# Attention over 48 heads: a deeper software pipeline, a fourth buffer for q and k, half of v's split on another engine

## The reference

```python
def rmsnorm(x, g):
    return x / np.sqrt(np.mean(x * x, axis=-1, keepdims=True) + 1e-06) * g
# q, k, v: (4, 12, 448, 64) float32
scores = (1 / sqrt(64)) * rmsnorm(q, g_q) @ rmsnorm(k, g_k).T      # 448 x 448, for each of 48 heads
attn = exp(scores - max); attn /= attn.sum() + 1e-9
x = (attn @ v) as (1792, 768)
# then: top-1 routing of the 1792 rows over 8 experts (cosine logits / tau),
# two matmuls per expert (768 -> 1024 -> 768), and a dense feed-forward 768 -> 2048 -> 768
```

## Time and profile before

| | us |
|---|---|
| three runs, median | 1331.34 |
| the profiled execution, its own time | 1328.66 |
| its span on the core | 1326.9 |
| attention: start to the first row sums of routing | 0 to 386 |
| of it the fill, up to the first head's `copy_u` | 34.9 |
| of it 48 heads, first to last `copy_u` | 348.1 |
| routing | 386 to 408 |
| experts and feed-forward | 408 to 1326.9 |

### The profile page before, as it was taken

The page is one execution under the profiler, slowest core; times in us unless marked ns, Lnnn a source line. Parts: engine busy times, 40 slices in busy tenths (PEclk is TensorE's granted clock), DMA queues, the critical chain, the costliest instruction groups (busy, mean ns, idle before and its releaser), DMA issues. The chain is left out here.

```text
span 1326.9 us, 21193 instructions
## 1 busy us (share of the span) xinstructions
PE 1232.0 (93%) x6986; PEld 1072.3 (81%) x6986; DVE 891.8 (67%) x1305; ACT 751.0 (57%) x1434; POOL 529.2 (40%) x533
## 2 busy tenths in 40 slices
PE   5988999999955999999999995999999999999998
PEld 3766777777744889998899985899999999999997
DVE  4877888888874999999999994455432235552222
ACT  4888888888873878777787774322241122221111
POOL 6666767676713776677766661000000000000000
PEclk9999999999986999999999997899999999999999
DMA  1233233322201355555555104121132222211222
GB/s 49 67 94 96 84 93 94 92 59 70 58 15 36 120 225 190 185 191 190 192 215 184 61 24 133 46 60 49 63 111 58 86 72 69 73 51 44 57 87 71
DMA packets 99979, 126.45 MB, mean 95 GB/s; under 512 B 28568, under 2 KB 81048, under 8 KB 99872
## 3 DMA queue, kind: packets, MB, share of 16 engines
q1 hardware_dynamic: 92416, 103.07, 25.6%
q0 software_dynamic: 3360, 16.52, 3.4%
q10 hardware_dynamic: 4096, 5.51, 1.2%
HBM read 193.88 MB, written 19.27 MB: 161 GB/s over the span
## 5 line engine op out<-in xcount | busy, mean ns | idle before, releaser
L1017 ACT CAST w_hi<-w_raw 128x768 fp32r<-128x768 f32 (+1 forms) x294 | 249.4, 930 | 15.2 <-DMA w_raw<-moe_w_in 13.9
L1087 DVE TENSOR_TENSOR w_lo<-w_raw,w_hi 128x1024 fp32r<-128x1024 f32 x84 | 187.9, 2272 | 9.7 <-POOL w_lo L906 7.0
L408 DVE TENSOR_TENSOR pT_lo<-ps_pt,pT_hi 112x448 fp32r<-112x448 f32 x192 | 115.1, 620 | 66.5 <-ACT pT_hi L354 66.3
L345 ACT ACTIVATE probs<-ps_s,neg_max 112x448 f32<-112x448 f32 x192 | 124.4, 648 | 45.1 <-DVE neg_max L402 45.1
L1497 DVE TENSOR_TENSOR out_lo<-out_raw,out_hi 128x384 fp32r<-128x384 f32 x64 | 35.7, 558 | 169.4 <-ACT out_hi L1406 169.4
L1288 PE MATMUL ps_acc<-yT_hi,in_hi 128*128 128x448 f32 x384 | 142.5, 371 | 2.1 <-DVE yT_lo L1483 2.1
L1318 PE MATMUL ps_acc<-gT_hi,out_hi 128*128 128x448 f32 x384 | 142.5, 371 | 0.0
L906 POOL TENSOR_TENSOR w_lo<-w_raw,w_hi 128x1024 fp32r<-128x1024 f32 x42 | 105.2, 2505 | 93.0 <-ACT w_hi L1017 93.0
L1289 PE MATMUL ps_acc<-yT_hi,in_lo 128*128 128x448 f32 x384 | 141.5, 369 | 0.0
L1290 PE MATMUL ps_acc<-yT_lo,in_hi 128*128 128x448 f32 x384 | 141.4, 368 | 0.0
L1320 PE MATMUL ps_acc<-gT_lo,out_hi 128*128 128x448 f32 x384 | 140.4, 366 | 0.0
(11 more groups left out here) (184 smaller groups left out, 2935.0 us busy)
## 6 DMA issues: line engine op xcount, KB each, us to landing
w_raw<-moe_w_in SPq DMA_DIRECT2D x84, 1536.0 KB
in_raw<-moe_w_in_in SPq DMA_DIRECT2D x32, 384.0 KB, 3.3
out_raw<-moe_w_out_in SPq DMA_DIRECT2D x64, 192.0 KB, 2.4
qk_raw<-q_in SPq DMA_DIRECT2D x48, 112.0 KB, 2.8
qk_raw<-k_in SPq DMA_DIRECT2D x48, 112.0 KB, 2.8
v_raw<-v_in SPq DMA_DIRECT2D x48, 112.0 KB, 2.0
x_rows<-x_tok SPq DMA_DIRECT2D x48, 112.0 KB, 2.5
out_rows<-o_sb ACTq DMA_DIRECT2D x26, 168.0 KB, 2.4
```

The lines of the kernel that those rows point to most:

```text
L345: act.activation(probs[:, t, :], ps_s[0:R, t, 0:S], ACT.Exp, bias=neg_max[u][:, t:t + 1], accum_out=sums[u][:, t:t + 1]).then_inc(s_exp, 1)
L1017: act.copy(out[:, c, :], raw[:, c, :]).then_inc(s_hi, 1)
L1087: dve.tensor_tensor(w1_lo[:, c, :], w1_raw[:, c, :], w1_hi[:, c, :].bitcast(F32), ALU.subtract).then_inc(s_w1lo, 1)
```

## The change

- The orders of the loops of PE, ACT, DVE and POOL are new, and each loop mixes steps of more heads. PE's iteration m now starts with transpose_p 1 (m) and runs values (m-1) on either side of transpose_p 2 (m); transposes of q are for head m+2, of k for m+3, scores g1 for m+1, g0 for m+2. ACT squares head m+4, POOL folds head m+5.
- `qk_raw` has four buffers instead of three: q and k of head n wait for the norms of head n-4.
- `v` of head n is issued by SP behind q and k of head n+5, and the store of head n behind q and k of head n+9 (LAG 9, V_LAG 5).
- The high part of v is made by POOL (`high_v`, a tensor_copy) instead of ACT. It comes first in POOL's iteration; `guard_sums` and `fold_squares` stand between it and the low part. `norm_q` and `norm_k` of a head now come one iteration after its `invert_rms`.
- `mix` holds 12 blocks instead of 48 (heads of the four batches share them), so that the copies that fill it once at the start are shorter.

The core of the diff:

```diff
-    LAG = 6
+    LAG = 9
+    V_LAG = 5
...
-        qk_raw = [sb(f"qk_raw{w}", [R, 2, T, D]) for w in range(3)]
+        qk_raw = [sb(f"qk_raw{w}", [R, 2, T, D]) for w in range(4)]
...
-        mix = sb("mix", [P, N, X])
+        mix = sb("mix", [P, H, X])
...
+            def load_qk(n):
+
+                if n > 3:
+                    sp.wait_ge(s_qn, n - 3)
+                    sp.wait_ge(s_kn, n - 3)
...
+            def load_v(n):
                 if n > 1:
                     sp.wait_ge(s_vhl, n - 1)
...
+            def step(n):
+                if n < N:
+                    load_qk(n)
+                if 2 <= n - V_LAG < N:
+                    load_v(n - V_LAG)
+                if 0 <= n - LAG < N:
+                    store(n - LAG)
...
+            def high_v(n, u):
+                pool.wait_ge(s_v_in[u], fills(n, u, 16))
+                if n > 1:
+                    pool.wait_ge(s_u, n - 1)
+                pool.tensor_copy(v_hl[u][:, :, 0, :], v_raw[u][:, :, :]).then_inc(s_vhi, 1)
```

More of the change, by code:

```diff
@@ L79, in attention @@
         s_gain_in, s_gain = sem("s_gain_in"), sem("s_gain")
-        s_qk_in = [sem(f"s_qk_in{w}") for w in range(3)]
+        s_qk_in = [sem(f"s_qk_in{w}") for w in range(4)]
         s_v_in = [sem(f"s_v_in{u}") for u in range(2)]
@@ L107, in store @@
                 sp.dma_start(x_dest[:, :, bass.ds(n * D, D)], x_tok[:, :, bass.ds(n, 1), 0:D].rearrange("p t o d -> p t (o d)")).then_inc(s_x_out, 16)
[L109 to L120, removed]
+            def step(n):
[5 more added lines that the diff above has]
+                    store(n - LAG)
+            load_qk(0)
             for half in range(2):
@@ L123, in _ @@
                     sp.dma_start(gains[half * D:(half + 1) * D, i:i + 1], g.rearrange("(d o) -> d o", o=1)).then_inc(s_gain_in, 16)
-            load(1, 1)
+            load_qk(1)
             sp.dma_start(emb_sb[:, :], emb).then_inc(s_emb, 16)
             sp.dma_start(tau_b[:, :], tau.rearrange("(o t) -> o t", o=1).to_broadcast([E, 1])).then_inc(s_emb, 16)
[L127 to L134, removed]
+            for n in range(2, 4):
+                load_qk(n)
+            load_v(0)
+            load_v(1)
+            for n in range(4, N + LAG):
+                step(n)
+                if LAG < n <= LAG + 2 * (C1 + C2) and (n - LAG) % 2 == 0:
+                    c = (n - LAG) // 2 - 1
+                    w, raw = (w1, w1_raw[:, c, :]) if c < C1 else (w2, w2_raw[:, c - C1, :])
+                    c = c if c < C1 else c - C1
+                    sp.dma_start(raw, w[0, c * P:(c + 1) * P, :]).then_inc(s_first, 16)
         def fills(n, u, per):
@@ L278, in transpose_emb @@
                     last.then_inc(s_te, 1)
[L280 to L289, removed]
+            for m in range(-3, N + 1):
                 if 0 <= m < N:
                     transpose_p(m, m % 2, 1)
+                if 0 <= m - 1 < N:
+                    values(m - 1, (m - 1) % 2, 0)
+                if 0 <= m < N:
                     transpose_p(m, m % 2, 2)
+                if 0 <= m - 1 < N:
+                    values(m - 1, (m - 1) % 2, 1)
+                if 0 <= m + 2 < N:
+                    transpose_q(m + 2, (m + 2) % 2)
                 if 0 <= m + 1 < N:
-                    scores(m + 1, (m + 1) % 2, 0)
-                if m + 2 < N:
-                    transpose_k(m + 2, (m + 2) % 2)
+                    scores(m + 1, (m + 1) % 2, 1)
                 if 0 <= m < N:
@@ L299, in _ @@
                     transpose_p(m, m % 2, 3)
-                if m - 1 >= 0:
+                if 0 <= m + 1 < N:
+                    transpose_p(m + 1, (m + 1) % 2, 0)
+                if 0 <= m - 1 < N:
                     outputs(m - 1, (m - 1) % 2)
+                if 0 <= m + 3 < N:
+                    transpose_k(m + 3, (m + 3) % 2)
+                if 0 <= m + 2 < N:
+                    scores(m + 2, (m + 2) % 2, 0)
         @block.scalar
@@ L373, in _ @@
                 if 0 <= m + 1 < N:
[L374 to L379, removed]
-                    copy_q(m + 1, (m + 1) % 2)
[L381 to L387, removed]
+                    copy_q(m + 1, (m + 1) % 2)
+                if 0 <= m - 2 < N:
+                    copy_u(m - 2, (m - 2) % 2)
         @block.vector
```

100 lines of the change are left out of this document (45 added, 55 removed).

## The result

The changed kernel takes 1275.22 us (median of four runs, 1275.01 to 1277.84) against 1331.46 of the kernel before in its four. The ratio is 0.9584, 95% interval 0.9562 to 0.9605: 56 us less. The forecast was 1290, with 1277 as its low end, so the mechanism and the sign were right and the gain was sized at 38 us instead of 54 on the profiled execution. That execution's own time is 1275.01 us, its span 1273.3. One run in this document, of the kernel before with the fourth buffer and v behind q and k, took 1725.86 us at a granted clock of 0.654, where the five others of that kernel had 0.971 to 0.976, and is left out of its number.

A forecast was written before the change was run, and what follows sets the result against it. A ring of waits between ACT and DVE was taken to bound attention. New attention 307.2 us less 348.1 now, plus 2.4 for fill, gives -38.5 on 1328.66: 1290.2, given as 1290; range 1277 to 1312.

The forecast's parts named there:

- The next bound is PE's list itself: Attention loop: under the new orders no ring through ACT and DVE is as long as PE's own work, 6.55 us a head.
- 6.55 us for that list, and 6.6 a head: PE in attention: work summed from start distances to 6.56, taken as 6.55, plus 0.05 us for small waits.
- Each change costs a tenth more or less: PE: uncertainty per change between transposes and products, giving 6.4 to 6.7 us a head.
- The ring of the kernel before: Attention: ACT and DVE wait for each other through low part 1 and row maxima, setting 7.36 us a head.
- v on POOL: High part of v: ACT loses 0.41 us a head, POOL gains a copy of 0.45 (0.20 to 0.74); zero price.
- q and k four heads ahead: Loads with the fourth buffer: the square's stall goes; priced nothing, at worst the 0.05 us a head remains.
- Fill: Start of attention up to the first `copy_u`: 37.3 instead of 34.9 us, +2.4, with 0 and +6 as ends.
- Drain: End of attention: last two iterations lack steps of heads that do not exist; 10.2 us up to the last `copy_u`.
- (1): Attention: ring shorter but not gone, 6.8 to 7.2 us a head, 1299 to 1317; chance 0.19.
- (2): Attention: PE has less work than its spacing says and DVE binds, 6.1 us a head, 1268; chance 0.07.
- (3): Attention: POOL binds from a copy of 1.4 us; 1344 at 2.6; chance 0.07 including other ways of losing.
- (4): No change within 0.3%: PE keeps waits of 0.8 us a head, for example for `ps_pt`; chance 0.05.

The follow-up runs named there:

- A shorter list: Changed kernel without the product of v with the low part of the probabilities (half of PE's matmuls of values): 1252.73 us, ratio 0.9431.
- the three orders: Changed kernel, on PE: outputs and k's transposes exchanged, 1276.89 us; transposes 1 and 2 side by side, 1279.48; q's beside them too, with DVE exchange, 1279.55.
- the runs with v on POOL: Kernel before with v's high part on POOL: 1327.96 us; the same plus fourth buffer and v issued behind q and k of three heads later: 1322.72.
- the runs above: Kernel before with fourth buffer and v issued behind q and k of three heads later: 1324.56 us, ratio 0.9952; with the buffer alone: 1329.74, 0.9997.

## Why the prediction was right and wrong, point by point

- **"The next bound is PE's list itself"**: right. A shorter list makes attention shorter by 23.8 us, and PE is busy in 200.00 of 200 us, which alone would not show it. The plan's waits came as written down: ACT waits for PE's transposes 2 (31 times, up to 0.4 us; 0.6 was read) and for nobody else.
- **6.55 us for that list, and 6.6 a head**: this is the step that failed, a term sized too long in a mechanism that was right. Measured is 6.39, in four orders 6.38 to 6.39. The 6.56 was pieced together from start distances of one early head of the kernel before; the head shown above adds up to 6.40. Of the 0.16 between them 0.07 is a step priced by its likeness: the last part of the probabilities was taken at 0.44, as the transposes of k, and is 0.37 ahead of values (204.41 to 204.78). Another 0.05 are the two halves of values, 0.93 and 0.91 there, 0.90 and 0.89 here. The other steps differ by their neighbours, up and down: outputs 0.85 ahead of scores and 0.75 ahead of k, q 0.12 ahead of values and 0.28 ahead of scores. Why the old head's distances came out longer stays open; waits too short to be listed are likely, and aren't shown. With 0.05 on top for waits that didn't come it is 45 x 0.21 = 9.4 us. These alone would have given 1281, still in the range.
- **"Each change costs a tenth more or less"** as the bound of that term: wrong in kind, as the three orders show. It was the reason for 6.4 as a low end, where 6.4 was the value.
- **The ring of the kernel before**: it is there, but the claim that ACT's and DVE's handovers alone set 7.36 was incomplete. A second ring through PE had the same length, and the runs with v on POOL show it. For the forecast it made no difference, as the plan of the new order was checked against every wait in the code, not against the one ring.
- **v on POOL**: the copy is 0.405 us, in the range of 0.20 to 0.74 and near the 0.45 taken:

```profile
L153 POOL CAST v_hl<-v_raw 112x256 fp32r<-112x256 f32 x32 | 13.0, 405 | 0.0
```

  From start to start it costs 0.35 here (203.40 to 203.75 in the trace of the changed kernel). The advice of the Trainium skill (GPSIMD Engine Reference, Engine selection) against elementwise work on that engine has no weight in the new order: with the copy on ACT or on POOL attention takes the same time.
- **q and k four heads ahead**: the stall is gone as said, no square waits in full pipeline. The prediction saw in the buffer the 2.3 us of late heads, net of the drain (the runs above give 5 to 6); in the new order its absence costs 24.8. The forecast's sum doesn't change by it, but whoever ranks the parts of the change by that price leaves out the one that carries it.
- **Fill**: +2.4 us was forecast, +0.2 came (35.1 against 34.9). PE was taken at its lower speed up to iteration 1. The scores of the new fill show it at full speed from 25.4 on, 0.53 and then 0.36 for matmuls of the same shape, where before it came at 31.7. k of head 3 was there about when it was said (its transposes start at 30.28, 29.7 was put down), but iteration 1 starts at 31.87 and not at 34.5. Why the speed rose earlier isn't shown: from 17 to 25 us PE is busy 6.62 us in the new fill and 6.38 in the old.

```profile
25.07 0.53 PE L232 MATMUL ps_s<-kT_lo,qT_hi 64*112 64x448 f32 x2
25.44 0.36 PE L232 MATMUL ps_s<-kT_hi,qT_lo 64*112 64x448 f32 x2
```

- **Drain**: the last heads take 5.68, 5.07 and 4.05 us from copy to copy, 1.8 us less than was put down.
- **The sum of the misses**: 9.4 for the list and the waits, 1.8 for the drain, 2.2 for the fill, 1.7 behind attention: 15.1 of 1290.2 - 1275.0 = 15.2 us. The range missed by 1.8 us: with 6.4 a head it had 1281 and 4 us below that, and the other three, 5.7 us in sum, all went the same way. The last of them lies within what traces of the same code differ by (942.9 to 946.2 in the other kernels of the document), so that much is luck.
- **The rivals**: (1) no ring was left. (2) PE's list was indeed shorter than its spacing said, by 0.16 and not by 0.5. By the Trainium skill's rule on weight loads (Perfetto Trace Analysis, Identifying the Most-Contended Engine) PE would have had room: weight loads are busy 162.8 of 200 us, 81%. Here the runs don't agree: PE has no room, as the run with the shorter list shows. The matmul row is no proof of it either, since it reads 119.97 of 120 in that run too. (3) POOL binds at 0.94 us more than it has. (4) No wait of PE is left in the list.

## What to carry to other kernels

Before pricing a shorter step on one engine, look for a second ring that ties with the first: follow every wait of a period that ends within a tenth of a microsecond of another one, because the trace names only the later of the two. Start distances of single steps, taken from a kernel in which the engine waits, came out 0.16 us a head too long here; take such a sum as an upper bound, and give the range room for all its terms erring the same way. To show that an engine is the bound, make its list shorter and see the period follow: its busy row reads full in other cases too. A buffer's worth depends on the order around it: the fourth buffer was worth nothing alone, 6 us with v moved behind q and k, and 25 us in the new order.

## What the runs showed of the hardware

A run of transposes between products had no price of its own on PE: four, three or two runs a head gave 6.39, 6.39 and 6.38 us for the same instructions, although the start distance of a single step moved by up to 0.15 us with its neighbour. POOL takes 0.35 us from start to start for a plain copy of 112x256, 0.41 as the duration of one, against 0.74 for a subtraction of two such tiles. PE reached its full speed at 25.4 us in the new fill and at 31.7 in the old one, although the granted clock of both fills reads 1.00 from the start. In the trace of the kernel before with the fourth buffer alone it reads otherwise: 0.50 from 25 to 30 us and 1.00 from 35 on, and scores take 0.57 us there up to 28.4 and 0.36 to 0.37 from 33.5 on. The duration of an instruction isn't its cost: in the run with PE's list shorter, where ACT is busy 119.33 of 120 us, ACT's exps last 1.00 us in the mean against 0.68 in the changed kernel, at the same 0.62 from start to start.
